# Attention scores and P times V as 24 products of 32 queries each, where 8 products of 96 queries stood

## The chip, the core and the metric

The kernel runs on one core of a Trainium2 chip. The time is device time in microseconds of one execution, from the first to the last instruction of the program and what lies around it; lower is better. The engines that matter here are TensorE (PE: matrix products and transposes, with the load of the stationary operand shown apart as PEld), VectorE (DVE), ScalarE (ACT), GpSimd (POOL) and SyncE (SP), which issues all the transfers.

## The reference

Attention with a local context, followed by two feed-forward layers.

```
B, H, S, D = 4, 8, 768, 64;  chunk, left_ctx, right_ctx, n_mem = 32, 16, 8, 8
for c in range(24):                       # chunks of 32 queries
    k_full = [mem_k, k[c*32-16 : c*32+40]]        # at most 8 + 56 keys; v_full alike
    a = softmax(q_c @ k_full.T / 8)
    out[c] = a @ v_full
x = out as (3072, 512)
x = elu(x @ moe_w_in) @ moe_w_out         # 512 -> 2048 -> 512
h = maximum(x @ moe2_w_in, 0)
return (s * h*h + b) @ moe2_w_out
```

## The kernel before

**Attention.** The 3072 queries are cut into 32 units of 96 queries (three chunks) for all 8 heads. A unit's keys are the 120 of its context and the 8 of memory, 128 in all. Heads go in 4 pairs `j`, and `e` is the head within the pair. A head's 64 elements of q and k lie on SBUF partitions 0 to 63 (e = 0) or 64 to 127 (e = 1). For a unit n, TensorE does in this order: `transpose_k` (L963, 4 transposes), `transpose_q` (L972, 4), `score` (L984 and L990), `transpose_p` (L999, 8), `p_times_v` (L1015, 8 products).

`score(n)` first writes a mask into two PSUM banks, one for each e (L984: one product for a bank, with the chunks' permitted keys), and adds 8 products to it (L990). In each the stationary operand is the 96 queries of one head (64 partitions by 96), and the moving one its 128 keys. DVE then takes the maximum of all 8 heads (`maximum`, L1435), ACT the exponentials (`exps`, L1184), DVE the normalised P (`normalise`, L1448). In `p_times_v` the stationary operand is one head's V (128 keys by 64), and the moving one P transposed (128 keys by 96 queries). The result, 64 partitions by 96, goes to partitions 64e to 64e+63, and ACT copies it out (`place_x`, L1199 and L1204).

**Where a unit stands.** The first 17 units (`HEAD`) are a pipeline ahead of everything else, "the head" below. One iteration `it` on TensorE holds `score(it)`, the transposes of q and k of later units, idle products (L951, they keep the engine busy while it waits), `transpose_p(it-2)` and `p_times_v(it-3)`. `score(it)` waits for `P_ready` of the unit two before it, the semaphore that L1448 counts up. The other 15 units are woven into the first feed-forward layer, "the woven stretch": unit 17 begins before step 10 of this layer, and each next one 12 steps later (`WOVEN`). A step is 6 products of 128x128 by 512 (L1084 on the way up, L1099 on the way down).

**Feed-forward.** Both layers are seven-product (Strassen) block products, whose operands are split into a high and a low part. POOL prepares the weights in the first third of the time (L877, L849), ACT and DVE cut the activations (L1317, L1603). Each engine's order is the order in which its block writes it, and semaphores join them.

All attention products and transposes are in float32; the feed-forward products are in the reduced 4-byte type `float32r`.

Of the kernel before, what the change touches and what calls it, by code (L numbers as in the profile page):

```python
# [15 lines left out]
B, H, S, D = 4, 8, 768, 64  # L16
CHUNK, LEFT, RIGHT, MEM = 32, 16, 8, 8
QU = 3 * CHUNK
CTX = QU + LEFT + RIGHT
KEYS = CTX + MEM  # L20
# [239 lines left out]
def placed(n):  # L260
    return n + 1 + (n >= FIRST_X0)
# [30 lines left out]
def build(nc, q, k, v, mem_k, mem_v, w_in0, w_out0, w_in1, w_out1, s_in, b_in, out):  # L292
# [8 lines left out]
    with ctx:  # L301
# [30 lines left out]
        PT = [at.rearrange("p (e j t) -> p e j t", e=2, j=PAIRS) for at in (att[:, 4096:4864], att[:, 1024:1792])]  # L332
        qT = [at.rearrange("p (j t) -> p j t", j=PAIRS) for at in (att[:, 4864:5248], att[:, 1792:2176])]
        kT = [at.rearrange("p (j t) -> p j t", j=PAIRS) for at in (att[:, 5248:5760], att[:, 2176:2688])]
# [32 lines left out]
        def v_of(n):  # L367
            return v_first_at[n % AHEAD] if n < HEAD else v_nat

        def slot_of(n):  # L370
            return n % 2 if n < HEAD else 0
# [16 lines left out]
        def pairs(b, rows, width):  # L388
            return ps[0:rows, b, 0:PAIRS * width].rearrange("p (j t) -> p j t", j=PAIRS)

        def s_bank(n):
            return 2 * ((n + HEAD) % 2) if n < HEAD else 6
# [13 lines left out]
        def X_bank(n):  # L406
            return pairs(6, 128, QU)
# [540 lines left out]
        def _(pe):  # L948
# [27 lines left out]
            def score(n):  # L976
                if n < HEAD and n >= 2:
                    pe.wait_ge(P_ready, n - 1)
                pe.wait_ge(qT_sb, n + 1)
                pe.wait_ge(kT_sb, n + 1)  # L980
                i = slot_of(n)
                seen = may_see[:, {0: 0, UPB - 1: 1}.get(n % UPB, 2), :]
                for e in range(2):
                    nc.tensor.matmul(pairs(s_bank(n) + e, QU, KEYS), chunk_of[:, :],  # L984
                                     seen.unsqueeze(1).to_broadcast([3, PAIRS, KEYS]), start=True, stop=False,
                                     skip_group_check=True)
                for j in range(PAIRS):
                    for e in range(2):
                        half = slice(64 * e, 64 * e + 64)
                        last = nc.tensor.matmul(pairs(s_bank(n) + e, QU, KEYS)[:, j, :], qT[i][half, j, :],  # L990
                                                kT[i][half, j, :], start=False, stop=True, skip_group_check=True)
                last.then_inc(scores, 1)

            def transpose_p(n, e):
# [8 lines left out]
            def p_times_v(n):  # L1003
                if n < HEAD:
                    pe.wait_ge(v_first[n % AHEAD], 32 * (n // AHEAD + 1))
                    if n:
                        pe.wait_ge(x_placed, placed(n - 1))
                else:
                    pe.wait_ge(v_in, 32 * (n - HEAD + 1))
                pe.wait_ge(PT_sb[0], n + 1)  # L1010
                pe.wait_ge(PT_sb[1], n + 1)
                for j in range(PAIRS):
                    for e in range(2):
                        h = 2 * j + e
                        last = nc.tensor.matmul(X_bank(n)[64 * e:64 * e + 64, j, :], v_of(n)[:, h * D:(h + 1) * D],  # L1015
                                                PT[slot_of(n)][:, e, j, :], start=True, stop=True)
                last.then_inc(pv_done, 1)

            def piece(n, at):
                if at == K_T:  # L1020
                    transpose_k(n)
                elif at == Q_T:
                    transpose_q(n)
                elif at == SC:
                    score(n)
                elif at == P_T:
                    transpose_p(n, 0)
                    transpose_p(n, 1)
                elif at == PV:
                    p_times_v(n)  # L1030
# [89 lines left out]
            for it in range(-2, HEAD):  # L1120
                if it == 0:
                    pe.wait_ge(mask_done, 8)
                if it >= 0:
                    score(it)
                if 0 <= it + 1 < HEAD and it != 0:
                    transpose_q(it + 1)
                if it >= 3:
                    pe.wait_ge(PT_sb[0], it - 2)
                    idle_products(2, bank[4])
                else:  # L1130
                    idle_products(4, bank[6])
                if it >= 2:
                    transpose_p(it - 2, 0)
                    transpose_p(it - 2, 1)
                if it == 0:
                    transpose_k(1)
                    transpose_q(1)
                if it + 2 < HEAD and it != -1:
                    transpose_k(it + 2)
                if it >= 3:  # L1140
                    p_times_v(it - 3)
            pe.wait_ge(P_ready, HEAD - 1)
            step(0)
            transpose_p(HEAD - 2, 0)
            transpose_p(HEAD - 2, 1)
            p_times_v(HEAD - 3)
            step(1)
            transpose_p(HEAD - 1, 0)
# [574 lines left out]
```

## Time and profile before

| | |
|---|---|
| median of 3 runs | 1121.03 us (1120.98 to 1121.4) |
| the profiled execution, its own time | 1121.61 us |
| its span | 1119.7 us |
| TensorE busy | 1090.9 us, 97% of the span |
| VectorE, ScalarE, GpSimd busy | 830.9, 790.0, 343.4 us |

The span is what the trace covers; 1.9 us of the profiled execution's own time lie around it. "PE" rows are TensorE's matmuls, "PEld" rows its weight loads, which run beside them. A matmul's recorded duration holds the time in the pipeline, so consecutive ones overlap in the records, and what one costs the engine is read from the distance between starts.

### The profile page before, as it was taken

What the parts mean: (1) busy time and instruction counts of PE and PEld (TensorE: products, weight loads), DVE (VectorE), ACT (ScalarE), POOL (GpSimd) and SP (SyncE); (2) the same over time, 40 slices, a digit from 0 to 9 for tenths busy, and PEclk for the clock granted to TensorE, in tenths of its full rate; (3) what the DMA queues carried; (4) which work ended last, traced back from release to release, by engine and by line L of the source; (5) the groups of instructions that cost most, each with busy time, mean ns of one, the idle gap of its engine ahead of it and who ended that gap; (6) DMA issues with size and microseconds to landing.
All of it is one profiled execution on the core that took longest, in us unless ns stands there. A gap on an engine that the chain in (4) does not pass through costs nothing.

```text
span 1119.7 us, 18242 instructions
## 1 busy us (share of the span) xinstructions
PE 1090.9 (97%) x5787; PEld 871.0 (78%) x5787; DVE 830.9 (74%) x1240; ACT 790.0 (71%) x1866; POOL 343.4 (31%) x373
## 2 busy tenths in 40 slices
PE   8999999999999999999999999999999999999998
PEld 5777677766777777787887887888888888888886
DVE  5895798479977746988968968869657578566485
ACT  4997877786777657668768677587676476774574
POOL 5343787577123333104465032761000000000000
PEclk9999999999999999999999999999999999999999
DMA  9966868778798998979899698997696666776664
GB/s 196 199 123 205 259 177 262 221 222 257 205 281 246 263 266 242 311 238 390 282 356 339 194 334 308 356 336 243 204 308 198 189 193 199 217 216 190 194 198 152
DMA packets 195990, 273.44 MB, mean 244 GB/s; under 512 B 111928, under 2 KB 120120, under 8 KB 195896
## 3 DMA queue, kind: packets, MB, share of 16 engines
q1 hardware_dynamic: 195896, 272.28, 78.5%
q8 instruction: 47, 0.77, 0.3%
q14 instruction: 47, 0.39, 0.1%
HBM read 196.74 MB, written 75.50 MB: 243 GB/s over the span
## 4 chain that ended last, share of the span: by engine, by line
PE 80%; ACT 6%; DVE 6%; issue 4%; DMA 2%; POOL 1%; SPq 0%; ACTq 0%; DVEq 0%; POOLq 0%
PE ps L1099 37%; PE ps L1084 32%; PE ps L990 3%; ACT ps L1184 2%; PE ps L984 1%; DMA w_ring<-w_scratch 1%; ACT elu L1277 1%; PE ps L1015 1%; PE ps L999 1%; PE ps L951 1%; DVE g_lo L1603 1%; DVE att L1448 1%; PE ps L972 1%; ACT elu L1282 1%; PE ps L1042 1%
## 5 line engine op out<-in xcount | busy, mean ns | idle before, releaser
L1084 PE MATMUL ps<-xc_hi,w_ring 128*128 128x512 f32 x1248 | 400.1, 394 | 2.8 <-ACT s L1250 1.0
L1099 PE MATMUL ps<-g_hi,w_ring 128*128 128x512 f32 x1248 | 389.5, 393 | 8.3 <-DVE g_lo L1603 3.4
L1099 PEld LDWEIGHTS ps<-g_hi,w_ring 128*128 128x128 f32 x1248 | 232.1, 189 | 61.4 <-issue 4.4
L1084 PEld LDWEIGHTS ps<-xc_hi,w_ring 128*128 128x128 f32 x1248 | 234.3, 188 | 56.0 <-ACT s L1250 1.5
L1099 PE MATMUL ps<-g_lo,w_ring 128*128 128x512 f32 x624 | 243.9, 391 | 0.0
L1084 PE MATMUL ps<-xc_lo,w_ring 128*128 128x512 f32 x624 | 243.0, 389 | 0.0
L1603 DVE TENSOR_TENSOR g_lo<-X,g_hi 128x512 fp32r<-128x512 f32 x240 | 178.2, 748 | 22.5 <-ACT g_hi L1317 21.9
L1317 ACT ACTIVATE g_hi<-X 128x512 fp32r<-128x512 f32 x240 | 150.3, 630 | 59.2 <-PE ps L1099 55.2
L849 POOL TENSOR_TENSOR w_raw<-w_raw 128x256 fp32r<-128x256 f32 x100 | 99.4, 999 | 260.6 <-ACT w_raw L1335 260.6
L1517 DVE TENSOR_TENSOR X<-s,ps 128x512 f32<-128x512 f32 x96 | 65.6, 684 | 105.3 <-ACT s L1250 92.2
L1099 PEld LDWEIGHTS ps<-g_lo,w_ring 128*128 128x128 f32 x624 | 117.4, 188 | 24.9
L1084 PEld LDWEIGHTS ps<-xc_lo,w_ring 128*128 128x128 f32 x624 | 117.3, 188 | 22.6
L1184 ACT ACTIVATE ps<-ps,nbias 96x128 f32<-96x128 f32 x256 | 84.8, 331 | 11.8 <-DVE nbias L1435 11.6
L1603 DVE TENSOR_TENSOR g_lo<-T,g_hi 128x512 fp32r<-128x512 f32 x96 | 72.0, 756 | 23.7 <-ACT g_hi L1317 23.3
L1317 ACT ACTIVATE g_hi<-T 128x512 fp32r<-128x512 f32 x96 | 60.4, 629 | 29.9 <-PE ps L1099 29.3
L1598 DVE TENSOR_TENSOR X<-X 128x512 f32<-128x512 f32 x96 | 76.6, 812 | 5.6 <-ACT X L1303 5.4
L1303 ACT ACTIVATE X<-X,sb_scalars 128x512 f32<-128x512 f32 x96 | 75.6, 808 | 3.3 <-DVE X L1578 3.3
L1242 ACT ACTIVATE s<-ps 128x512 f32<-128x512 f32 x72 | 42.9, 596 | 48.2 <-PE ps L1084 41.7
L1236 ACT ACTIVATE ps<-ps 128x512 f32<-128x512 f32 x72 | 42.0, 584 | 46.0 <-PE ps L1084 40.9
L877 POOL TENSOR_TENSOR w_ring<-w_raw,w_ring 128x256 fp32r<-128x256 f32 x64 | 59.8, 944 | 32.1 <-ACT w_ring L1335 31.5
L1282 ACT ACTIVATE elu<-elu 128x512 f32<-128x512 f32 x96 | 59.2, 630 | 0.4
L1435 DVE TENSOR_REDUCE nbias<-ps 96x8 f32<-96x1024 f32 x32 | 39.0, 1218 | 23.8 <-PE ps L990 23.4
(165 smaller groups left out, 1528.5 us busy)
## 6 DMA issues: line engine op xcount, KB each, us to landing
w_ring<-w_scratch SPq DMA_DIRECT2D x280, 512.0 KB, 4.4
w_scratch<-w_raw SPq DMA_DIRECT2D x100, 256.0 KB, 5.4
w_scratch<-w_ring SPq DMA_DIRECT2D x64, 256.0 KB, 3.3
w_raw<-in_moe_w_in SPq DMA_DIRECT2D x16, 512.0 KB, 5.1
w_raw<-in_moe_w_out SPq DMA_DIRECT2D x16, 512.0 KB, 6.3
w_scratch<-w_later SPq DMA_DIRECT2D x24, 256.0 KB, 3.0
x_scratch<-y SPq DMA_DIRECT2D x12, 512.0 KB, 5.8
att<-x_scratch SPq DMA_DIRECT2D x12, 512.0 KB, 6.3
```

Source lines behind the costliest of these rows:

```text
L849: nc.gpsimd.tensor_tensor(lo, src, hi.bitcast(F32), ALU.subtract).then_inc(w_lo_done, 1)
L877: nc.gpsimd.tensor_tensor(lo, src, hi.bitcast(F32), ALU.subtract).then_inc(w_lo_done, 1)
L1084: last = nc.tensor.matmul(bank_of(st, st.i), w[:, a, cols], x[:, st.pi, kk, :], start=(st.pi in (P1, P5) and kk == 0 and n == 0), stop=(kk ...
L1099: last = nc.tensor.matmul(bank_of(st, d), w[:, a, cols], x[:, k % RING, :], start=(st.pi in (P1, P5) + (P4,) * (1 - st.gr) and st.i == 0 a ...
L1184: last = nc.scalar.activation(S_of(n)[:, h, :], S_of(n)[:, h, :], ACT.Exp, bias=nbias[:, i, h:h + 1], accum_out=rowsum[:, i, h, 0:1])
L1242: nc.scalar.activation(s2[:, i, :], acc_e[i][:, :], ACT.Copy).then_inc(s2_done, 1)
L1282: nc.scalar.activation(elu[:, m % 4, :], elu[:, m % 4, :], ACT.Exp, scale=-1.0).then_inc(exp_of_h, 1)
L1303: nc.scalar.activation(h, h, ACT.Identity, scale=sb_scalars[:, 0:1], bias=sb_scalars[:, 1:2]).then_inc(affine_done, 1)
L1317: nc.scalar.activation(g_hi[:, k % RING, :], g_raw(st), ACT.Copy).then_inc(g_hi_done, 1)
L1517: nc.vector.tensor_tensor(to, a, b, ALU.add).then_inc(done, 1)
L1598: nc.vector.tensor_tensor(to, a, b, ALU.subtract).then_inc(t_done, 1)
L1603: nc.vector.tensor_tensor(g_lo[:, k % RING, :], g_raw(st), g_hi[:, k % RING, :].bitcast(F32), ALU.subtract).then_inc(g_lo_done, 1)
```

## The change

In `score`, each of the 8 products is cut along the queries into three of 32. Each has a stationary operand of 64 partitions by 32 queries, the same 128 moving keys, and an output on its own 32 partitions of the bank. In `p_times_v`, each of the 8 products is cut along the moving operand: the same stationary V (128 by 64), 32 queries moving, into the same 64 output partitions at other columns. The semaphore is still counted up by the last product alone, and nothing else is changed. Every other engine has the same instructions in the same order.

```diff
                 for j in range(PAIRS):
-                    for e in range(2):
-                        half = slice(64 * e, 64 * e + 64)
-                        last = nc.tensor.matmul(pairs(s_bank(n) + e, QU, KEYS)[:, j, :], qT[i][half, j, :],
-                                                kT[i][half, j, :], start=False, stop=True, skip_group_check=True)
+                    for c in range(QU // CHUNK):
+                        for e in range(2):
+                            half, own = slice(64 * e, 64 * e + 64), slice(CHUNK * c, CHUNK * c + CHUNK)
+                            last = nc.tensor.matmul(pairs(s_bank(n) + e, QU, KEYS)[own, j, :], qT[i][half, j, own],
+                                                    kT[i][half, j, :], start=False, stop=True, skip_group_check=True)
                 last.then_inc(scores, 1)
...
                 for j in range(PAIRS):
                     for e in range(2):
                         h = 2 * j + e
-                        last = nc.tensor.matmul(X_bank(n)[64 * e:64 * e + 64, j, :], v_of(n)[:, h * D:(h + 1) * D],
-                                                PT[slot_of(n)][:, e, j, :], start=True, stop=True)
+                        for c in range(QU // CHUNK):
+                            own = slice(CHUNK * c, CHUNK * c + CHUNK)
+                            last = nc.tensor.matmul(X_bank(n)[64 * e:64 * e + 64, j, own], v_of(n)[:, h * D:(h + 1) * D],
+                                                    PT[slot_of(n)][:, e, j, own], start=True, stop=True)
                 last.then_inc(pv_done, 1)
```

On TensorE in the head, one iteration of the program stands as follows, before (-) and with the change (+). `s` is one of the buffers in which a unit's q and k lie, `att` holds P, and the shape is that of the output; `x8` is eight products in a row.

```order
-L999 MATMUL ps<-ident,att 128x96 x8
+L1000 MATMUL ps<-ident,att 128x96 x8
 L963 MATMUL ps<-ident,s 128x128 x4
-L1015 MATMUL ps<-att,X 64x96 x8
-L984 MATMUL ps<-may_see,chunk_of 96x512 x2
-L990 MATMUL ps<-att 96x128 x8
+L1018 MATMUL ps<-att,X 64x32 x24
+L984 MATMUL ps<-may_see,chunk_of 96x512 x2
+L991 MATMUL ps<-att 32x128 x24
 L972 MATMUL ps<-ident,s 128x96 x4
```

No row moves against another; the two groups of 8 become groups of 24 (line numbers behind them shift by up to 3).

On TensorE in the woven stretch, where unit 18's product with V stands between two steps on the way down, before:

```order
L1099 MATMUL ps<-g_hi,w_ring 128x512 x2
L1099 MATMUL ps<-g_lo,w_ring 128x512
L1015 MATMUL ps<-att 64x96 x8
L963 MATMUL ps<-ident,att 128x128 x4
L1099 MATMUL ps<-g_hi,w_ring 128x512 x2
```

and with the change:

```order
L1102 MATMUL ps<-g_hi,w_ring 128x512 x2
L1102 MATMUL ps<-g_lo,w_ring 128x512
L1018 MATMUL ps<-att 64x32 x24
L963 MATMUL ps<-ident,att 128x128 x4
L1102 MATMUL ps<-g_hi,w_ring 128x512 x2
```

Here too only the group's own row differs; the steps around it and the next unit's first transposes (L963) keep their places.

## Rows read from the trace of the kernel before

**Rows 1.** The page, busy time and share of each engine

```profile
PE 1090.9 (97%) x5787; PEld 871.0 (78%) x5787; DVE 830.9 (74%) x1240; ACT 790.0 (71%) x1866; POOL 343.4 (31%) x373
```

**Rows 2.** The page, shares of the chain that ended last

```profile
PE 80%; ACT 6%; DVE 6%; issue 4%; DMA 2%; POOL 1%; SPq 0%; ACTq 0%; DVEq 0%; POOLq 0%
```

**Rows 3.** Stretches: length, busy time and count of each engine, clock, DMA

```profile
51.44:56.00 4.56, 4.53 (x52) 3.43 (x52) 4.38 (x8) 4.53 (x21) 0.00 (x0) 1.00 1.09 216
60.00:80.00 20.00, 18.97 (x223) 14.19 (x220) 18.79 (x29) 19.12 (x88) 8.34 (x6) 1.00 0.66 127
80.00:92.00 12.00, 10.24 (x108) 7.38 (x108) 10.76 (x19) 11.16 (x49) 2.93 (x2) 1.00 0.13 34
130.00:200.00 70.00, 65.02 (x354) 49.60 (x354) 61.35 (x80) 51.75 (x147) 56.02 (x57) 0.98 0.71 224
200.00:300.00 100.00, 93.25 (x549) 70.97 (x549) 79.29 (x114) 75.39 (x206) 59.92 (x64) 1.00 0.79 237
300.00:400.00 100.00, 97.67 (x554) 76.24 (x554) 77.11 (x121) 72.55 (x199) 30.91 (x27) 1.00 0.86 252
```

**Rows 4.** The chain in order of time, one head iteration: start, us, what

```profile
51.44 0.63 PE ps L984 x2
52.07 1.05 PE ps L990 x16
53.12 0.48 PE ps L972 x4
53.60 0.43 PE ps L951 x2
54.03 0.66 PE ps L999 x8
54.69 0.47 PE ps L963 x4
55.16 0.81 PE ps L1015 x16
```

**Rows 5.** Groups by line, TensorE, whole run: busy us, mean ns

```profile
L990 PE MATMUL ps<-att 64*96 64x128 f32 x512 | 36.1, 281 | 0.0
L999 PE MATMUL ps<-ident,att 96*128 96x96 f32 x256 | 26.4, 246 | 0.2 <-ACT att L1193 0.2
```

**Rows 6.** L990 in short stretches: length, PE and PEld busy (instructions under way)

```profile
42.87:42.95 0.08, 0.08 (x2) 0.08 (x2) 1.00 1.44 173
42.95:43.05 0.10, 0.10 (x2) 0.10 (x4) 1.00 1.28 161
43.05:43.16 0.11, 0.11 (x4) 0.11 (x4) 1.00 2.08 310
```

**Rows 7.** TensorE in order of time, 49 to 51.5 us: start, duration

```profile
49.31 0.82 PE L999 MATMUL ps<-ident,att 96*128 96x96 f32 x8
49.97 0.63 PE L963 MATMUL ps<-ident,y 128*128 128x128 f32 x4
50.53 0.88 PE L1015 MATMUL ps<-att,X 128*64 128x96 f32 x16
```

**Rows 8.** Weight loads of L1015, first 60 ns of a group, in time

```profile
41.37 0.19 PEld L1015 LDWEIGHTS ps<-att,X 128*64 128x64 f32 x3 [0.17 <-issue]
```

**Rows 9.** Weight loads of L1015, first 50 ns of that group

```profile
41.37:41.42 0.05, 0.05 (x2) 1.00 1.36 210
```

**Rows 10.** TensorE's timeline at the head's end: waits in brackets

```profile
84.71 0.63 PE L984 MATMUL ps<-may_see,chunk_of 3*96 3x512 bf16 x2 [0.70 <-DVE att L1448]
89.28 0.50 PE L1084 MATMUL ps<-xc_hi,w_early 128*128 128x512 f32 x1 [0.76 <-DVE att L1448]
```

**Rows 11.** TensorE's timeline, score group of unit 19 in the woven stretch

```profile
162.66 1.12 PE L990 MATMUL ps<-att 64*96 64x128 f32 x16
163.71 0.73 PE L1099 MATMUL ps<-g_hi,w_ring 128*128 128x512 f32 x2
```

**Rows 12.** Waits of TensorE, 130 to 450 us: total, times, longest

```profile
PE ps L1099 <- DVE g_lo L1603: 4.1, 5, 1.8
PE ps L972 <- ACT att L1204: 3.6, 3, 1.7
PE ps L1099 <- POOL w_ring L877: 2.5, 1, 2.5
```

**Rows 13.** Around the one fall of the clock in the woven stretch

```profile
152.00:155.00 3.00, 3.00 (x9) 2.38 (x8) 3.00 (x6) 2.81 (x7) 2.42 (x2) 0.53 0.44 165
```

## The prediction

> **What bounds the kernel now.** I read four views: the page's busy times, the chain that ended last, stretches by stage, then TensorE's own instructions in the two groups that change. TensorE is busy 97% of the span [rows 1] and carries 80% of the chain [rows 2]. So time added to TensorE costs time, except where it waits for another engine just then.
>
> The head has a period of 4.56 us an iteration, and from 51.44 to 56.00 TensorE is busy 4.53 of it, ACT 4.53, DVE 4.38 [rows 3]. The chain's seven pieces of that iteration are all TensorE's [rows 4] and add up to 4.53 us. So in the head TensorE time goes to the end one for one. Its last part is different: of 60 to 92 us TensorE is idle for 1.03 and 1.76 us [rows 3], with waits for DVE's normalised P of 0.70 us before the last mask product and 0.76 us before step 0 [rows 10]. In the woven stretch it is idle for 4.98, 6.75 and 2.33 us from 130 to 400 us, 14.1 us together [rows 3], for DVE, ACT and POOL [rows 12].
>
> **What one product costs today.** The score group takes 1.05 us in the chain [rows 4]; in the woven stretch it is 1.05 us again from its start to the next step's [rows 11]. 
>
> What are the two of a pair? Transposes alone on the array tell. Eight of 96 columns last 0.82 us with a tail of 246 ns, so one is (0.82 - 0.246) / 7 = 82 ns [rows 5, 7], and four of 128 columns, with the tail of L990's records (281 ns, their mean [rows 5]), (0.63 - 0.28) / 3 = 117 ns [rows 7]. The 16 records of P times V, also 96 columns, last 0.88 us: less the tail 0.246 and the first load 0.05 it is 0.58 over 7 steps, 83 ns a step [rows 7]. So one record needs the same time alone (transposes) as two records need together (products). Two passes of one product can't both use one part of the array in that time. The likelier reading is that the two heads e = 0 and 1, on separate halves of the array (rows 0 to 63 and 64 to 127 for scores, columns for P times V), run side by side, the second head's first pass ahead of the first head's second pass.
>
> **The change, part by part.**
>
> *Scores.* Eight products of 128 moving columns become 24 of the same 128 columns: 16 more per unit. On six separate parts (2 halves of rows by 3 groups of 32 columns) each part has 4 products of 2 passes, 8 passes of 0.109 us = 0.87 us, as now. The first load has 32 columns in place of 96 (about -0.05), the six parts start one behind the other (about +0.03 by the pairs' distance). I take 0. The other bound is that no more than a pair is ever side by side, 24 steps in place of 8: 16 x 0.109 = +1.74 us. I take 0 because the trace already shows parts overlapping both along rows (scores) and along columns (P times V); the distance is that six at once are not shown.
>
> *P times V.* The moving part falls from 96 to 32 columns, a third of 83 ns: 28 ns. But V is loaded anew for each product. Of a group's weight loads two have started after 50 ns and three after 60 ns [rows 8, 9]; the third waits for the first, so a load of 64 columns takes about 55 ns, and sets the pass. Each half has 12 products of 2 passes: 24 x 0.055 = 1.32 us against 8 x 0.083 = 0.66 now, **+0.66 us**. Lower bound: loads hide wholly, 24 x 0.028 = 0.67 us, +0. Upper bound: in the new order one head's three products follow each other on the same half; if the other half isn't reached past them, it is 48 x 0.055 = 2.64 us, +1.98. I take +0.66, since pairs show that a pass can overtake.
>
> So a unit costs +0.66 us of TensorE. Nothing else changes: DVE, ACT, POOL and SP keep all instructions, and who waits for `scores` (the maximum L1435, with all of DVE's later work behind it) waits no longer if the scores cost nothing more; who waits for the product with V is ACT's L1199 or L1204, one iteration ahead of its need in the head, while in the woven stretch the next unit's L972 waits for it and is then late by the same 0.66 us as TensorE itself.
>
> *The sum.* Head: 17 x 0.66 = 11.2 us. In its last part DVE and ACT set the period, and TensorE's idle time takes some: of 1.03 + 1.76 us I let 2.1 be used, +9.1. Woven: 15 x 0.66 = 9.9. The waits are spread over 270 us in bursts, and TensorE's addition helps only where it stands before one and doesn't itself delay the engine waited for; I let a quarter go, 2.5 us, +7.4. Ends: nothing taken, +9.9, or all of it within the 14.1 us of idle time, 0. Together +16.5 us on the profiled 1121.61, 1138.1; the runs shown have their median 0.58 lower, so **1137.5 us**. The likeliest case by itself reaches from 1130 (woven part free) to 1148 (nothing taken, and some 0.3 us a unit in which 96 weight loads and matmuls must be issued in 0.9 us, twice and more today's rate of 32 in 0.66).
>
> That issue bound has a page beside it. The Trainium skill ("TensorE: Matmul & The Clock Gate", Part 1) says that starts of matmuls are never closer than about 25 ns, however small they are. By it 48 matmuls of a score group would need 1.2 us, an estimate of +0.33 us a unit and +10 us in all; the pairs of rows 6 start closer than that, so it doesn't hold for separate parts here.
>
> **The rivals.**
>
> *In order, two at a time.* What speaks for it: nothing in the trace shows more than a pair, and another reading of the pair is that it is one product's own two passes, with the heads one behind the other. Then scores cost +1.74 and P times V +0.66, 2.40 a unit. Head 17 x 2.40 - 2.1 = 38.7; woven 36.0 less a quarter = 27.0; +65.7, **1186.7 us**. Against it: a pair takes the time of one lone record. The same skill page, Part 3, says that matmuls start and end strictly in program order, also between parts. With it an overtaking pass isn't possible and this rival is what follows; the time of rows 7 speaks against the page, since no order of whole passes in line gives 8 steps for 16.
>
> *P times V serial, scores free.* Three products of a head in a row hide the other half: 1.98 a unit, head 33.7 - 2.1, woven 29.7 x 0.75, +53.9, **1175 us**. Both together are 3.72 a unit, 61.1 + 41.9 = +103, **1224 us**.
>
> *Not slower.* A load of V that is already in the array costs nothing, or loads run ahead on both halves so that the group stays at 0.66 us. It decides at a product with V of 28 ns a pass; above some 30 ns the kernel is slower. Then the time is **1121 us**, and 1119.5 if the clock's fall goes away: from 152 to 155 us the granted clock is 0.53 [rows 13], behind the wait of 2.5 us for POOL [rows 12], and three-odd us at half clock cost some 1.7 us. For it: a shorter wait there. Against it: the third load's start [rows 8, 9].
>
> *The clock.* In the head it is at its full level, 2.4 GHz (1.00) [rows 3]; parts of a quarter of the array or less may let it fall to 1.2 GHz. Against it: transposes and today's half-size products fill the head and it stays. A fall through the head would cost up to 40 us.
>
> **How the numbers follow.** Measured differences under 0.2% (2.2 us) can't be told from none. Six parts at once 0.42 (1130 to 1148); in order, two at a time 0.28 (about 1187, 1178 to 1194); P times V serial 0.11 (1175); both 0.07 (1224); not slower 0.06 (0.03 of it faster); the clock or something unseen 0.06. The predicted time is the first case's. The range of 1128 to 1191 holds the first, third and most of the second. Slower 0.94, same 0.03, faster 0.03.
>
> **What would show it.** Head iterations of 5.2 us (6.96 by the second case, 6.5 by the third). The score group in the chain still about 1.05 us (2.8 if in order), with more than eight of its records under way at once in 0.1 us. P times V about 1.47 us from 0.81 [rows 4], its loads 55 ns apart for each half. The 130 to 400 us stretches with less idle TensorE time, and everything behind 450 us of the same length, only later. I am wrong if the score group grows by more than 0.1 us, if the product with V takes 2.6 us, or if the woven stretch grows by more or less than 7 to 10 us.

## The result and the profile after

The changed kernel takes 1140.7 us (median of 4 runs, 1139.1 to 1142.32), against 1121.01 for the one before: a ratio of 1.017, 95% interval 1.0155 to 1.0186. The profiled execution took 1139.1 us, the fastest of the four; its span is 1137.1, 17.4 more than before. The rows of the changed kernel are of this execution.

The page's first row, busy time of each engine, stands against [rows 1]. TensorE has 24 us and 2048 matmuls more, and no other engine more than 0.6 us:

```profile
PE 1115.1 (98%) x7835; PEld 898.1 (79%) x7835; DVE 830.7 (73%) x1240; ACT 790.6 (70%) x1866; POOL 343.8 (30%) x373
```

One head iteration in the chain (start, us, what), as [rows 4]:

```profile
55.54 0.56 PE ps L984 x2
56.10 1.02 PE ps L991 x48
57.12 0.48 PE ps L972 x4
57.60 0.43 PE ps L951 x2
58.03 0.66 PE ps L1000 x8
58.70 0.44 PE ps L963 x4
59.14 1.66 PE ps L1018 x48
```

Two things stand in these rows. The score group holds 48 records in 1.02 us, where 16 took 1.05. P times V went from 0.81 to 1.66 us. The period is 5.25 us.

TensorE's weight loads and matmuls of one score group in short stretches (length, PE busy with those under way, PEld busy), as [rows 6]:

```profile
56.10:56.16 0.06, 0.06 (x6) 0.06 (x12) 1.00 0.99 278
56.17:56.27 0.10, 0.10 (x12) 0.10 (x11) 1.00 1.16 279
56.28:56.38 0.10, 0.10 (x18) 0.10 (x10) 1.00 1.26 294
```

Where two were added at a step, it is six now: 6, 12, 18 under way, at the same distance of 0.109 us. The group's first matmul starts at 56.03, and a window of 0.04 us from there already holds all six:

```profile
56.03:56.07 0.04, 0.04 (x6) 0.04 (x8) 1.00 1.09 333
```

So the six parts of the array work side by side.

The stages of the changed kernel, as [rows 3]: a head iteration, three pieces of the woven stretch, and all behind it.

```profile
55.54:60.79 5.25, 5.25 (x118) 4.25 (x118) 4.38 (x8) 4.64 (x22) 0.00 (x0) 1.00 1.08 224
140.00:210.00 70.00, 65.95 (x537) 51.40 (x533) 59.93 (x78) 51.00 (x146) 54.16 (x56) 0.98 0.70 219
210.00:310.00 100.00, 95.61 (x818) 73.79 (x817) 79.61 (x113) 75.41 (x206) 62.82 (x65) 1.00 0.76 231
310.00:410.00 100.00, 98.08 (x835) 77.19 (x834) 74.09 (x116) 70.70 (x195) 25.77 (x23) 1.00 0.84 243
469.00:1137.00 668.00, 661.28 (x2952) 544.34 (x2950) 488.64 (x734) 450.88 (x817) 127.53 (x135) 1.00 0.77 256
```

And the last stage of the kernel before, from 17 us earlier and 1 us shorter:

```profile
452.00:1119.00 667.00, 660.49 (x2946) 543.17 (x2944) 488.21 (x731) 450.45 (x814) 126.14 (x134) 1.00 0.77 256
```

Behind the woven stretch nothing changed by more than 1 us: TensorE is idle for 6.7 us there, and was for 6.5. Where the 17.4 us came about shows in the starts of two products with V, the last of the head (unit 16) and the last of all (unit 31). TensorE's timeline of the kernel before:

```profile
99.22 0.88 PE L1015 MATMUL ps<-att,X 128*64 128x96 f32 x16
441.31 0.88 PE L1015 MATMUL ps<-att 128*64 128x96 f32 x16
```

and with the change:

```profile
108.42 1.73 PE L1018 MATMUL ps<-att,X 128*64 128x32 f32 x48
458.77 1.73 PE L1018 MATMUL ps<-att 128*64 128x32 f32 x48
```

The head is 9.2 us later, the woven stretch adds 8.3, 17.5 together. The last product's own +0.85 lies behind these starts; of the 18.3 us at its end, 0.9 are made up by the end of the span.

### The profile page after: what moved, and what is told of

Read it like the earlier page. It is cut to its first block, busy times and chain, and to the rows that moved or that the text cites. A ratio compares the mean times of both kernels' runs of the same rounds, so it can differ in the third digit from the quotient of the medians.

```text
span 1137.1 us, 22338 instructions
## 1 busy us (share of the span) xinstructions
PE 1115.1 (98%) x7835; PEld 898.1 (79%) x7835; DVE 830.7 (73%) x1240; ACT 790.6 (70%) x1866; POOL 343.8 (30%) x373
## 4 chain that ended last, share of the span: by engine, by line
PE 85%; ACT 4%; DVE 4%; issue 2%; DMA 2%; SPq 2%; POOL 0%; ACTq 0%; DVEq 0%; POOLq 0%
PE ps L1102 37%; PE ps L1087 35%; PE ps L1018 4%; PE ps L991 3%; PE ps L1000 1%; ACT ps L1187 1%; PE ps L984 1%; DMA w_ring<-w_scratch 1%; DVE g_lo L1606 1%; PE ps L963 1%; PE ps L972 1%; PE ps L1045 1%; ACT elu L1280 1%; ACT elu L1285 1%; DVE X L1572 1%
```

## The experiments

**Each half of the change alone.** The first run has the diff of `score` alone, the second that of `p_times_v` alone.

> Only the scores are cut into 24 products; P times V has its 8 products of before. Theory A (six parts of the array work side by side, and the whole loss is P times V's weight loads): score group of 48 records still 1.0 us in the chain, head iteration 4.5 to 4.6 us, the time 1120 to 1122 us, no difference from before that 5 rounds can tell. Rival B (the cut scores also cost, by the change of mode or by issue, and P times V hides part of it): head iteration above 4.6 us, 1123 us or more.

1122.22 us (11 runs) against 1121.94, ratio 1.0005 (0.9994 to 1.0017). A head iteration, as a stretch, and the score group in the chain:

```profile
51.36:55.93 4.57, 4.52 (x84) 3.35 (x85) 4.38 (x8) 4.52 (x21) 0.00 (x0) 1.00 0.77 178
```

```profile
51.98 1.08 PE ps L991 x48
```

Three times the products, the same period and the same time. The piece of 1.08 us here goes on to DVE; in the kernel before such pieces of the score group are 1.07, and those that go on to TensorE 1.05. Theory A holds, B falls.

> Only P times V is cut into 24 products; the scores have their 8 of before. Theory A: head iteration 5.25 to 5.35 us, P times V 1.66 us in the chain, the time 1138 to 1142 us, all of the loss. Rival B (scores share the loss): below 1136 us.

1142.06 us (4 runs, 1138.68 to 1146.26), ratio 1.0181 (1.0155 to 1.0206). In its chain:

```profile
50.99 1.05 PE ps L990 x16
54.05 1.66 PE ps L1017 x48
```

The ranges of this run and of the changed kernel overlap: all of the loss is P times V's, as far as these runs can tell.

**The order of P times V.** Both groups cut, and the two halves of the array in turn:

```diff
                 for j in range(PAIRS):
-                    for e in range(2):
-                        h = 2 * j + e
-                        for c in range(QU // CHUNK):
+                    for c in range(QU // CHUNK):
+                        for e in range(2):
...
```

> Both groups cut, but in P times V the two halves of the array take turns (chunk loop outside the head loop), where one head's three products stood in a row. Theory C (the second half starts about 0.14 us late, because the first half's six passes stand ahead of it, and otherwise each half runs its 24 passes at 58 ns): P times V 1.66 to about 1.53 us, head iteration 5.12, the time 3 to 4 us below the changed kernel, 1136 to 1138. Rival D (the order of issue doesn't matter, the sum of loads does): 1139 to 1142. Rival E (with halves in turn both load at the full rate and hide under each other): P times V near 0.9 us, 1122 to 1125.

1137.13 us (1136.43 to 1138.32), ratio 1.0136 (1.0122 to 1.015), against 1.017 of the changed kernel. The group in the chain:

```profile
53.68 1.52 PE ps L1017 x48
```

The weight loads tell why. The changed kernel, from the group's start to 59.19 and 59.25 us (start, duration, how many loads have begun):

```profile
59.06 0.25 PEld L1018 LDWEIGHTS ps<-att,X 128*64 128x64 f32 x3 [0.17 <-issue]
59.06 0.31 PEld L1018 LDWEIGHTS ps<-att,X 128*64 128x64 f32 x5 [0.17 <-issue]
```

and with the halves in turn, to 53.74 and 53.80:

```profile
53.60 0.26 PEld L1017 LDWEIGHTS ps<-att,X 128*64 128x64 f32 x6 [0.17 <-issue]
53.60 0.31 PEld L1017 LDWEIGHTS ps<-att,X 128*64 128x64 f32 x8 [0.17 <-issue]
```

From there on both add two loads every 0.06 us. But after 0.13 us the changed kernel has begun three, one behind the other, where it is six with the halves in turn. A record doesn't name its half; the starts of the matmuls fall into two chains of 24, each with 58 ns from one to the next, and in the changed kernel the second chain starts 0.14 us behind the first and ends as late. Theory C holds; its size was right.

**How far ahead a part takes up its work.** Only the scores cut, in another order:

```diff
-                for j in range(PAIRS):
-                    for c in range(QU // CHUNK):
-                        for e in range(2):
+                for e in range(2):
+                    for j in range(PAIRS):
+                        for c in range(QU // CHUNK):
...
```

> Only the scores cut, and all 12 products of e = 0 stand ahead of all 12 of e = 1. Each of the three parts of a half then has 8 passes in a row. Theory F (a part takes up its work however far ahead in the program it stands): score group 1.0 to 1.1 us, time as before. Rival G (reach is short, a few passes of a part): e = 1 starts when e = 0 has about 4 of its 8 passes left, group about 1.4 to 1.5 us, head iteration 4.95, the time 8 to 12 us above before. Rival H (strict order beyond the next product): the group doubles to 1.9 us and the time rises by some 22 us.

1131.99 us, one run, 10 above the median of the kernel before on the same chip. Its score group in the chain, and in short stretches:

```profile
52.26 1.51 PE ps L991 x48
```

```profile
52.26:52.62 0.36, 0.36 (x12) 0.36 (x15) 1.00 1.09 208
52.66:52.75 0.09, 0.09 (x12) 0.09 (x9) 1.00 0.64 117
53.02:53.12 0.10, 0.10 (x18) 0.10 (x5) 1.00 0.87 156
53.24:53.34 0.10, 0.10 (x12) 0.10 (x5) 1.00 1.00 328
```

Up to 52.62 only e = 0 works, three parts of four passes. From 52.66 on both halves work, and when e = 0 has done its eight, e = 1 has four left. The group has 12 steps where it had 8. Rival G holds: a part takes up work about four passes deep, and what stands further on waits although its part of the array is free.

That the depth belongs to each part, and is no reach shared by all, follows from this run and the changed kernel together. By the starts of the records e = 1 begins here as the fifth of eight passes on each part of e = 0 has begun; in P times V of the changed kernel it begins as the third of six passes has (0.138 and 0.144 us into the group). Three passes of a part are still to start both times, but nine in all here and three there.

**What sets a pass of P times V.** Three runs, each on the one with the halves in turn:

```diff
# 64 queries moving, overlapping
-                            h, own = 2 * j + e, slice(CHUNK * c, CHUNK * c + CHUNK)
+                            h, own = 2 * j + e, slice(16 * c, 16 * c + 64)
# half a load (half of the output is left out)
-  X_bank(n)[64 * e:64 * e + 64, j, own], v_of(n)[:, h * D:(h + 1) * D]
+  X_bank(n)[64 * e:64 * e + 32, j, own], v_of(n)[:, h * D:h * D + 32]
# 16 products of 48
-                    for c in range(QU // CHUNK):
+                    for c in range(2):
-                            h, own = 2 * j + e, slice(CHUNK * c, CHUNK * c + CHUNK)
+                            h, own = 2 * j + e, slice(48 * c, 48 * c + 48)
```

> As the run with the halves in turn, but each of the 24 products with V moves 64 queries in place of 32 (they overlap, and write the same values again): the same loads, twice the moving work. Theory A (a pass is as long as the load of V's 64 columns, 58 ns): 64 columns move in 64 x 0.83 + 3 = 56 ns, still hidden, so P times V stays at 1.52 to 1.55 us and the time at 1136 to 1139. Rival I (the moving part or the sum of load and moving sets the pass): a pass grows by 27 ns, P times V to 2.15 us, the time to some 1153.

> As the run with the halves in turn, but each product with V loads only 32 of a head's 64 columns of V (half of the output is left out): the same number of loads and products, each load half as long. Theory A: a pass is about 30 ns, P times V 0.85 to 0.95 us, head iteration near 4.6, the time 1121 to 1125. Rival J (the number of instructions sets the pass): 1.52 us and 1137 as before it.

> As the run with the halves in turn, but P times V in 16 products of 48 queries. Theory A: 48 columns move in 43 ns, so the load of 58 ns still sets each of the 16 passes of a half: P times V 16 x 0.058 + 0.12 = 1.05 us, 0.24 over the kernel before, the time 1126 to 1129. Rival J (by the number of instructions) gives about the same; rival I (load and moving add up) 1.5 us and 1136.

Measured: 1137.28 us (ratio 1.013, 1.0104 to 1.0155), 1124.81 (1.0022, 1.0006 to 1.0038) and 1126.41 (1.0037, 1.0023 to 1.0051). The group in the chain of each, first with 64 columns moving:

```profile
53.03 1.55 PE ps L1017 x48
```

then with half the load:

```profile
50.49 0.88 PE ps L1017 x48
```

and with 16 products:

```profile
50.89 1.07 PE ps L1017 x32
```

Twice the moving columns cost 0.03 us; half the load takes 0.64 us away at the same number of instructions. The pass is as long as the load of V, 58 ns. With half the load it is some 31 ns. Rivals I and J fall. The group is back near its old 0.81 only when the load shrinks; what else the cut may cost is within the 0.07 us that are left.

**A version that could win.** If parts work side by side, scores by chunk have a use: a chunk sees 64 of the 128 keys, and needs only these as moving columns. The first try keeps the layout (the edit in outline):

```diff
-                    kT[i][half, j, :]                      # 128 keys
+  for lo, hi in ((CHUNK * c, seen_at), (CTX, KEYS)) if seen_at < CTX else ((CHUNK * c, KEYS),):
+                    kT[i][half, j, lo:hi]                  # 56 and 8, or 64
```

> P times V as in the kernel before, scores cut by chunk, and each chunk multiplied only with the 64 keys that it may see (56 in a row and the 8 of memory; for the first two chunks these are two products, 56 and 8 columns). The other columns keep the mask alone, the result is the same. A part then has 4 times 2 passes of 56 columns (49 ns) and 2 of 8 (a load of 32 columns, about 30 ns), 0.63 us, against 0.87. Theory K (six parts side by side, TensorE bounds the woven stretch and ACT the head at 4.53 us): score group 0.75 to 0.85 us, head unchanged, 15 x 0.25 less in the woven stretch, 1117 to 1119. Rival L (more passes than a part may hold ahead, so the parts come out of step): group 1.0 us or more and no gain.

1124.72 us (12 runs), ratio 1.0018 (1.0003 to 1.0033), barely slower. TensorE's timeline of one unit (the row names the shape of its first records; the idle time before a row is in brackets):

```profile
51.95 1.06 PE L993 MATMUL ps<-att 64*32 64x56 f32 x80
55.64 0.49 PE L972 MATMUL ps<-ident,y 96*128 96x96 f32 x4 [2.63 <-issue]
```

80 passes take about as long as 16 long ones did: 0.95 us in the chain where 0.75 to 0.85 was expected, 12 ns for a pass with its load. Whether a rate of handing out sets this, or rival L, no run settles. And the profile shows one stall of 2.63 us in which TensorE waits for no engine. The iteration with the stall takes 7.96 us and the one behind it, most of it at a granted clock of 0.50, takes 6.36; the head's steady iterations take 4.49, less than the 4.56 before. So in this execution the loss in the head is the stall and the clock, not the cut itself.

The second try, in outline too, lays the memory keys in the middle, so each chunk's keys are one stretch and 24 products do; `SEEN` is ((0, 64), (32, 96), (56, 128)), and `cuts` the three chunks' queries with these keys:

```diff
-  k: rows of the context to [0:120], memory to [120:128]     # v alike, the mask too
+  k: the first 56 rows to [0:56], memory to [56:64], the other 64 to [64:128]
+                    for own, keys in cuts if n >= HEAD else [(slice(0, QU), slice(0, KEYS))]:
+                        for e in range(2):
+                            nc.tensor.matmul(pairs(...)[own, j, keys], qT[i][half, j, own], kT[i][half, j, keys], ...)
```

> All products as in the kernel before; only the 8 memory keys are laid between the 56th and the 57th key of the context, so that each chunk's keys lie in one stretch. That adds a transfer for k and one for v per unit. It is the control for the two runs beside it. Expected 1120 to 1123 us: the loads of the head run several units ahead of their use. Rival: the head's transfers, its engines full until some 66 us, come late, 1125 or more.

> The same layout, and in the 15 woven units alone the scores are cut by chunk, each with the 64 to 72 keys in a row that it may see: 24 products, 8 passes of at most 72 columns on each of six parts, 8 x 0.063 = 0.51 us in place of 0.87. Theory K (six parts side by side, and the woven stretch is TensorE's): score group 0.65 to 0.7 us from 1.05, 15 x 0.38 = 5.7 us less TensorE work, of which a quarter or so falls into waits: 4 to 5.7 us below the control, 1115.5 to 1118. Rival L (more instructions cost what the columns save): group above 0.9 us and no measurable gain.

> As the run beside it, with the scores of the head's 17 units cut too. Theory K and M (the head is bound by ACT at 4.53 us an iteration once TensorE has less to do, and 17 x 64 more instructions in it can run the instruction stream dry, as one stall of 2.6 us showed in the run with 40 products): no gain over the cut in the woven units alone, from 0.5 us better to 3 us worse, 1115 to 1121. Rival N (the head is TensorE's own): another 17 x 0.38, 1110 to 1112.

Control 1123.18 us (ratio 1.0008, 0.9999 to 1.0016), cut in the woven units 1121.68 (1.0, 0.9987 to 1.0013), cut everywhere 1122.47 (1.0, 0.9989 to 1.0012). Both cut kernels missed the times expected, 1115.5 to 1118 and 1115 to 1121. The group of a woven unit in the chain, control and cut:

```profile
431.01 1.05 PE ps L999 x16
```

```profile
429.46 0.69 PE ps L1001 x45
```

The products do what they should, -0.36 us in each of 15 units, 5.4 us. The medians show 1.5 of it, which is within their spread; the spans of the two profiled executions, 1123.3 and 1123.1 us, show 0.2. Two stretches of these, 130 to 200 and 200 to 300 us, show where some of the rest went (length, PE, PEld, DVE, ACT, POOL, granted clock, DMA); the control:

```profile
130.00:200.00 70.00, 64.61 (x361) 48.85 (x360) 63.11 (x79) 51.81 (x148) 55.24 (x55) 0.98 0.72 219
200.00:300.00 100.00, 92.81 (x540) 70.97 (x539) 78.23 (x113) 76.07 (x209) 61.88 (x68) 1.00 0.77 235
```

and the cut in the woven units:

```profile
130.00:200.00 70.00, 64.55 (x459) 49.37 (x458) 61.76 (x80) 51.66 (x147) 53.92 (x56) 0.95 0.72 223
200.00:300.00 100.00, 91.17 (x657) 69.34 (x656) 78.56 (x111) 74.78 (x205) 61.57 (x66) 0.98 0.76 229
```

TensorE's mean granted clock falls from 0.98 to 0.95 and from 1.00 to 0.98. 0.03 of 70 us and 0.02 of 100 are 4 us of full clock withheld, and in the second stretch TensorE also idles 1.6 us more; that about covers the 5.2 us missing between these two executions. One fall, at 244.6 us, stands right behind a wait of 2.17 us for ACT that the control doesn't have. Over all executions the clock takes less: its mean over the span is 0.9976 in the 29 of the kernel before, 0.9972 in the control's 11, 0.9959 in the 12 with the cut woven units and 0.9945 in the 12 cut everywhere. Against the control 0.0013 of 1122 us is 1.5 us, 0.0027 is 3.0. So less TensorE work came with less clock each time; how the one leads to the other isn't shown.

Cut everywhere, the head did get shorter. Its iterations take from 4.20 us up in that trace, in place of 4.56, so ACT with its 4.53 us doesn't bind them, and the last mask product starts at 83.07 us, at 86.32 with the cut in the woven units alone. The profiled execution loses that in one place, before a transpose in the woven stretch:

```profile
182.80 0.90 PE L981 MATMUL ps<-ident,att 96*128 96x96 f32 x4 [6.04 <-ACT att L1215]
```

From 182.1 to 188.9 us the granted clock is 0.50. Why ACT is that late there no run shows. No version beats the kernel before by a measurable amount.

## Why the prediction was right

The direction, the case and the time were forecast (1137.5, measured 1140.7, range 1128 to 1191), and the step on which all turned, six parts side by side, is shown by the count of records and by the scores alone at 1.0005. The range is wide, since it holds rivals too; that the time lies near the forecast is in part luck (see the sum). By its steps:

- **Who is bound.** Right for the changed kernel: TensorE is never idle in its steady iterations, which went from 4.56 to 5.25 us, forecast 5.2. For the kernel before it was read from one iteration, whose chain is all TensorE's. From 24 to 47 us the chain passes through DVE's normalised P (L1448) in every iteration, since the next mask product waits for it. From the chain of the kernel before, one round of 4.56 us: mask, scores, their maximum, the normalised P of the unit before (pieces of 0.02 us left out).

```profile
37.75 0.63 PE ps L984 x2
38.38 1.07 PE ps L990 x16
39.48 1.22 DVE nbias L1435
40.70 0.09 DVE total L1441
40.81 0.21 DVE rinv L1444
41.04 1.23 DVE att L1448
42.27 0.04 issue
```

  TensorE's own work in an iteration is less, 4.43 us: its pieces in the changed kernel, with P times V at 0.81 in place of 1.66 and the scores at 1.05 in place of 1.02. The loop also fits the period of other runs, by the length of their score group: 5.0 us with one half first (group 1.51), 4.49 with 80 passes (0.98), 4.20 at the least with the cut everywhere (0.69).
- **Scores, 0 us.** Right: 1.02 us in place of 1.05. The rival of strict order, 1187 us, falls with it: with one half of the scores ahead of the other, both halves' passes start in turn from 52.66 us on. The Trainium skill's rule beside it ("TensorE: Matmul & The Clock Gate", Part 3), that matmuls start strictly in program order, doesn't hold here either. Nor does the floor of about 25 ns between starts that the Trainium skill gives (same page, Part 1), between separate parts of the array: six matmuls start within 0.04 us [56.03 to 56.07]. The prediction took this from rows 6, whose windows of 0.08 us and more can't show it.
- **P times V, +0.66 us.** Right mechanism, too small: 1.66 against 0.81 in the chain, +0.85. A pass set by its load takes 58 ns and not 55 (24 of them make 0.07 us of it), and the second half starts some 0.14 us late, which the forecast treated as all or nothing; the halves in turn give 0.14 of it back.
- **What is absorbed.** Mis-sized as well, in the other direction. A unit costs +0.85 - 0.03 = 0.82 us of TensorE. Up to the start of unit 16's product with V stand 16 such products and 17 score groups, 16 x 0.85 - 17 x 0.03 = 13.1 us; the head grew by 9.2, so 3.9 were absorbed, where I let 2.1 be. The last part took 1.9 of it, near the 2.1. 9 iterations gave 0.13 each, 1.2 us: the difference between the loop's 4.56 and TensorE's own 4.43, which I took for work, since the chain's pieces of one iteration added up to 4.53. The first three iterations took 0.4. The other 0.4 isn't absorbed: the first mask product, ahead of all that the change cuts, starts at 8.42 us in place of 8.85. In the woven stretch it is 15 x 0.82 = 12.3, of which 8.3 show: 4.0 absorbed, a third and not a quarter. TensorE's idle time in the three windows is 4.05, 4.39 and 1.92 us, 10.4 in place of 14.1 [rows 3].
- **The sum.** +9.1 and +7.4 were forecast, 9.2 and 8.3 measured. The two terms are this near by luck, because two errors cancel: by the forecast's share of absorption and the measured price it would have been some +20 us. These rows are of the profiled execution, 1.6 us below the median. And the upper end of the likeliest case, 1148, doesn't follow from its own terms: with nothing taken and 0.3 us more a unit it is 1121 + 11.2 + 9.9 + 9.6, some 1152.
- **The clock.** It stayed at 2.4 GHz in the head (1.00), and the fall in the woven stretch stayed too (0.98 from 140 to 210 us). The price of up to 40 us for a fall through the head has no row in the prediction. The nearest is in the run with 80 passes: 6.36 us for an iteration most of which is at half clock, 4.49 for a steady one, some 32 us for 17 (an estimate from these two).

## What to carry to other kernels

Cutting small float32 products over separate parts of the array was free here with 48 passes in a group, since each part's chain of passes got no longer: count passes for each part, not products. With 80 passes that count no longer gave the time (0.95 us where 0.75 to 0.85 was expected). Where a cut repeats the load of the same stationary operand, compare the load with the moving columns; once the load is longer, every extra product costs its full load. Write the order so that the parts take turns, for the second part is reached only about four passes deep. Read what sets the period from several iterations, not from one: here a second loop, 3% longer than the engine's own work, decided what a saving or a cost was worth. And a few microseconds taken from TensorE came back as clock and waits here.

## What the runs showed of the hardware that I had not expected

- TensorE hands a part of the array its passes ahead of other parts' work that stands earlier in the program, but only about four deep: e = 1 started as the fifth of eight passes of e = 0 had begun (1.51 us in place of 1.05).
- Three parts across the columns and two across the rows make six float32 products at once; 48 records take 1.02 us, 16 take 1.05.
- 80 passes in a score group took 0.95 us in the chain, some 12 ns for a pass with its load; what sets that pace isn't shown.
- TensorE stood still for 2.63 us with no engine to wait for, in the head of the run with 80 passes a group, and for 1.16 us in the head of the one with half a load. Such a gap of 1.12 us stands in the kernel before too, at 282 us. What it waited for no run shows.
